# A second plain block that also makes the sums of weights; seven products in three blocks instead of four

## What is computed

```python
for t in range(S):
    state = gamma * state + einsum('bhd,bhe->bhde', k[:, :, t], v[:, :, t])
    y[:, :, t] = scale * einsum('bhd,bhde->bhe', q[:, :, t], state)
x = y as (3072, 512)
h = x @ w_in                      # 512 -> 2048
g = where(h >= 1, h, where(h <= -1, 0, (h + 1)**2 / 4))
x = g @ w_out                     # 2048 -> 512
h = x @ w_in2                     # 512 -> 1024
ln = layernorm(h * softmax(h)) * g_ln
out = ln @ w_out2                 # 1024 -> 512
```

## Time and profile before

| | |
|---|---|
| median of 3 runs | 903.12 us |
| the profiled execution | 901.88 us |
| span of its instructions | 900.1 us |
| mean granted TensorE clock | 0.979 of full |
| TensorE matmul busy | 855.7 us, 95% |
| VectorE busy | 578.3 us, 64% |
| ScalarE busy | 355.6 us, 40% |
| GpSimd busy | 270.9 us, 30% |

### The profile page before, as it was taken

The page is one execution under the profiler, slowest core; times in us unless marked ns, Lnnn a source line. Parts: engine busy times, 40 slices in busy tenths (PEclk is TensorE's granted clock), DMA queues, the critical chain, the costliest instruction groups (busy, mean ns, idle before and its releaser), DMA issues.

```text
span 900.1 us, 14076 instructions
## 1 busy us (share of the span) xinstructions
PE 855.7 (95%) x5392; PEld 729.3 (81%) x5392; DVE 578.3 (64%) x1046; ACT 355.6 (40%) x557; POOL 270.9 (30%) x244
## 2 busy tenths in 40 slices
PE   9978975999999998999989999999999999999998
PEld 7766764888888887888878887888877888888886
DVE  5677765554675457645575554367788889888841
ACT  3343332222242223322242223336466766767541
POOL 3534534222432234222431212224621311122000
PEclk9999996999999999999999999999999999999999
DMA  9944562443444343544333430421044465545452
GB/s 350 378 164 149 165 210 92 167 139 120 141 126 142 120 143 103 156 150 141 121 120 120 132 117 1 141 94 48 0 164 153 147 190 171 181 130 170 144 166 70
DMA packets 75587, 129.13 MB, mean 143 GB/s; under 512 B 7552, under 2 KB 25984, under 8 KB 75520
## 3 DMA queue, kind: packets, MB, share of 16 engines
q1 hardware_dynamic: 75232, 127.97, 43.9%
q10 hardware_dynamic: 288, 0.26, 0.1%
HBM read 94.65 MB, written 33.55 MB: 142 GB/s over the span
## 4 chain that ended last, share of the span: by engine, by line
PE 71%; DVE 15%; ACT 5%; issue 4%; SPq 2%; DMA 2%; POOL 1%; ACTq 0%; DVEq 0%; POOLq 0%
PE acc L622 22%; PE h L530 18%; PE o_ps L1399 13%; PE p L1299 10%; PE h L592 3%; DVE x_lo L874 2%; PE att L473 2%; DVE g_raw L963 2%; PE att L484 2%; ACT g_raw L740 1%; DMA w_pair<-in_moe_w_in 1%; DVE s_raw L889 1%; PE att L508 1%; DVE g_raw L958 1%; SPq L298 1%
## 5 line engine op out<-in xcount | busy, mean ns | idle before, releaser
L622 PE MATMUL acc<-g_hi,w 128*128 128x512 f32 x768 | 259.0, 398 | 0.0
L1091 POOL TENSOR_TENSOR g_lo<-g_raw,g_hi 128x512 fp32r<-128x512 f32 x96 | 129.1, 1344 | 364.4 <-ACT g_hi L665 364.4
L622 PEld LDWEIGHTS acc<-g_hi,w 128*128 128x128 f32 x768 | 145.1, 189 | 35.3 <-issue 3.6
L971 DVE TENSOR_TENSOR h<-h 128x256 f32<-128x256 f32 x192 | 81.1, 423 | 130.8 <-PE h L530 92.0
L740 ACT ACTIVATE g_raw<-g_raw,half_bias 128x512 f32<-128x512 f32 x96 | 69.2, 720 | 237.4 <-DVE g_raw L958 237.4
L622 PE MATMUL acc<-g_lo,w 128*128 128x512 f32 x384 | 150.5, 392 | 0.0
L530 PE MATMUL h<-x_hi,s 128*128 128x256 f32 x512 | 98.1, 290 | 0.9 <-DVE g_raw L963 0.9
L665 ACT ACTIVATE g_hi<-g_raw 128x512 fp32r<-128x512 f32 x96 | 60.7, 633 | 94.5 <-DVE g_raw L963 94.5
L530 PE MATMUL h<-x_hi,w 128*128 128x256 f32 x384 | 73.8, 288 | 20.2 <-DVE x_lo L874 12.5
L530 PEld LDWEIGHTS h<-x_hi,s 128*128 128x128 f32 x512 | 84.8, 198 | 3.6 <-DVE g_raw L963 1.2
L963 DVE TENSOR_TENSOR g_raw<-h,g_raw 128x512 f32<-128x512 f32 x96 | 68.8, 717 | 25.2 <-ACT g_raw L740 25.2
(11 more groups left out here) (140 smaller groups left out, 1512.2 us busy)
## 6 DMA issues: line engine op xcount, KB each, us to landing
s<-w_sums SPq DMA_DIRECT2D x128, 256.0 KB, 2.7
z<-zq SPq DMA_DIRECT2D x24, 512.0 KB, 2.8
zt<-z SPq DMA_DIRECT2D x94, 128.0 KB, 3.1
kT<-in_kT SPq DMA_DIRECT2D x24, 256.0 KB, 3.0
q<-in_q SPq DMA_DIRECT2D x24, 256.0 KB, 2.9
v<-in_v SPq DMA_DIRECT2D x24, 256.0 KB, 3.6
x2T<-y SPq DMA_DIRECT2D x24, 256.0 KB, 3.0
x_raw<-x2T SPq DMA_DIRECT2D x12, 512.0 KB, 4.9
```

The costliest lines, as they stand in the source:

```text
L622: last = mm(acc[m][:, :], ww, gg[:, f % 2, :], start=f == 0 and t == 0, stop=f == FT1 - 1 and t == 2)
L971: tt(out, of_product(p), other, ALU.add).then_inc(sem["taken1"], 1)
L1091: tt(g[1][:, f % 2, :], gate[:, f % 2, :], g[0][:, f % 2, :].bitcast(F32), ALU.subtract)\
```

## The change

Block 1 becomes a second plain block. The making of the sums of weights moves from block 0 to it, in steps 0, 1, 3, 4, 6, 7, 9 and 10 (the low parts in the steps after), and the SyncE queue is reordered to match; `store_x2(0)` stands in it ahead of the first `store_sums`. Blocks 2, 3 and 4 keep the seven products. In a pair, product 7 comes before product 6. `X_ORDER[0]`, the order of splits at the change to the first seven-product block, is t3, t2, t4, b11, b21, t1, b22. At the change from one seven-product block to the next, ScalarE copies b11 and b21 before it copies the high part of the previous activation; VectorE subtracts t3 after `larger` and no longer ahead of the joins of products 5 and 3; GpSimd makes t1 directly behind t3. At the change to block 5 (and to block 1) the four quarters of y are split by `split_y(blk, kt)` among the last step's work and no longer behind all of it.

```diff
-SEVEN = range(1, BLOCKS - 1)
+SUMS_BLOCK = 1
+SEVEN = range(SUMS_BLOCK + 1, BLOCKS - 1)
-P_ORDER = (1, 2, 6, 7, 5, 3, 4)
+P_ORDER = (1, 2, 7, 6, 5, 3, 4)
-PREPARE_AT = (2, 4, 5, 7, 8, 10, 11, 13)
+PREPARE_AT = (0, 1, 3, 4, 6, 7, 9, 10)
...
@@ SyncE @@
+            for c in range(B + 1, 2 * B + 1):
+                load_kT(c)
+                load_rest(c)
+            load_pair(0)
+            load_pair(1)
+            store_x2(0)
+            for b in range(B):
+                if b:
+                    load_kT(2 * B + b)
+                    load_pair(2 * b + 1)
+                    load_rest(2 * B + b)
+                store_sums(2 * b)
+                if b < B - 1:
+                    load_pair(2 * b + 2)
+                store_sums(2 * b + 1)
...
@@ TensorE, pair @@
+                have("t3")
+                product(7, sums(0), "t3")
                 have("t2")
-                product(6, sums(0), "t2")
-                have("t3")
-                product(7, sums(1), "t3")
+                product(6, sums(1), "t2")
...
@@ ScalarE, pair @@
+                if more:
+                    split_part(blk + 1, "b11")
+                    split_part(blk + 1, "b21")
                 if q:
                     high(*divmod(blk * FT1 + f - 1, FT1))
                 if more:
-                    for name in ("b11", "b21", "t3"):
-                        split_part(blk + 1, name)
+                    split_part(blk + 1, "t3")
+                if last:
+                    split_y(blk + 1, 0)
+                    split_y(blk + 1, 1)
                 square(blk, f)
+                if last:
+                    split_y(blk + 1, 2)
+                    split_y(blk + 1, 3)
...
@@ VectorE, pair @@
                 if more:
-                    for name in ("b11", "b21", "t3"):
-                        split_part(blk + 1, name)
+                    split_part(blk + 1, "b11")
+                    split_part(blk + 1, "b21")
                 join(q, 5, part, part, 3)
...
+                if last:
+                    split_y(blk + 1, 0)
                 larger(blk, f)
+                if last:
+                    for kt in range(1, KT):
+                        split_y(blk + 1, kt)
                 if more:
-                    split_part(blk + 1, "t2")
-                    split_part(blk + 1, "t1")
+                    for name in ("t3", "t2", "t1"):
+                        split_part(blk + 1, name)
...
@@ VectorE, dense: at the change to the first block with seven products @@
+                    if change:
+                        for name in X_ORDER[0][:4]:
+                            split_part(blk + 1, name)
                     clamp(blk, f)
+                    if change:
+                        split_part(blk + 1, X_ORDER[0][4])
                     larger(blk, f)
+                    if change:
+                        for name in X_ORDER[0][5:]:
+                            split_part(blk + 1, name)
-                    if blk == 0:
-                        if f in PREPARE_AT:
-                            sums_of_weights(PREPARE_AT.index(f))
+                    if blk == SUMS_BLOCK:
                         if f - 1 in PREPARE_AT:
                             sums_low(PREPARE_AT.index(f - 1))
+                        if f in PREPARE_AT:
+                            sums_of_weights(PREPARE_AT.index(f))
...
@@ GpSimd, pair @@
                 if more:
                     sum_of_x(blk + 1, "t3")
+                    sum_of_x(blk + 1, "t1")
                 if q:
                     low(*divmod(blk * FT1 + f - 1, FT1))
                 if more:
-                    sum_of_x(blk + 1, "t1")
                     sum_of_x(blk + 1, "t2")
```

More of the change, by code:

```diff
@@ L60, in made, with pair_number @@
     return len(P_ORDER) * q + P_ORDER.index(product) + 1
+def pair_number(blk, p):
+    return (blk - SEVEN[0]) * FPAIRS + p
 def h_count(blk, f):
-    return (FT1 if blk else 0) + f + 1
+    return min(blk, SEVEN[0]) * FT1 + f + 1
 def x_parts(blk):
-    return 0 if blk == 0 else 7 * blk if blk in SEVEN else 7 * len(SEVEN) + KT
+    return sum(7 if n in SEVEN else KT for n in range(1, blk + 1))
 X_ORDER = (("t3", "t2", "t4", "b11", "b21", "t1", "b22"), ("b11", "b21", "t3", "t2", "t1", "b22", "t4"))
 def x_made(blk, part):
-    return x_parts(blk - 1) + X_ORDER[min(blk - 1, 1)].index(part) + 1
+    return x_parts(blk - 1) + X_ORDER[min(blk - SEVEN[0], 1)].index(part) + 1
 def steps(blk):
@@ L580, in up @@
                 n = blk * FT1 + f
-                if blk and f < 2:
+                if blk > SEVEN[0] and f < 2:
                     pe.wait_ge(sem["taken1"], 7 * LAST_Q)
@@ L653, in _ @@
                 outputs(c)
-            dense(0)
+            for blk in range(SEVEN[0]):
+                dense(blk)
             for blk in SEVEN:
@@ L751, in dense @@
                 for f in range(steps(blk)):
-                    if blk == 0 and f == FT1 - 1:
-                        for name in X_ORDER[0]:
-                            split_part(1, name)
+                    if f == FT1 - 1 and blk + 1 < SEVEN[0]:
+                        for kt in range(KT):
+                            split_y(blk + 1, kt)
+                    if f == FT1 - 1 and blk + 1 == SEVEN[0]:
+                        for name in X_ORDER[0][:-1]:
+                            split_part(blk + 1, name)
                     if f == LAG - 1 and blk:
@@ L757, in dense @@
                     square(blk, f)
+                    if f == FT1 - 1 and blk + 1 == SEVEN[0]:
+                        split_part(blk + 1, X_ORDER[0][-1])
                     high(blk, f)
@@ L762, in dense @@
                         split_w_out(f)
[L763 to L764 removed]
+                    if blk == SUMS_BLOCK and f in PREPARE_AT:
+                        sums_high(PREPARE_AT.index(f))
                     if blk == BLOCKS - 1:
@@ L768, in pair @@
             def pair(blk, p):
-                q = (blk - 1) * FPAIRS + p
+                q = pair_number(blk, p)
                 f = 2 * p
                 more = blk + 1 in SEVEN and p == FPAIRS - 1
+                last = blk + 1 not in SEVEN and p == FPAIRS - 1
                 if p == 1:
@@ L872, in split_part, with split_y @@
                 if name == "t2":
-                    dve.wait_ge(sem["x_summed"], 4 * blk)
+                    dve.wait_ge(sem["x_summed"], 4 * (blk - SEVEN[0]) + 4)
                 tt(x_part(name, 1), x_raw(name), x_part(name, 0).bitcast(F32), ALU.subtract)\
                     .then_inc(sem["x_lo"], 1)
[L877 to L881, removed]
+            def split_y(blk, kt):
+                dve.wait_ge(sem["x_hi"], x_parts(blk - 1) + kt + 1)
+                tt(x[1][:, kt, :], y[:, kt, :], x[0][:, kt, :].bitcast(F32), ALU.subtract)\
+                    .then_inc(sem["x_lo"], 1)
             def sums_of_weights(i):
@@ L988, in pair @@
                 join(q, 7, part7, part, 2)
-                if p == 0 and blk > 1:
+                if p == 0 and blk > SEVEN[0]:
                     split_part(blk, "b22")
@@ L1018, in dense @@
                 for f in range(steps(blk)):
-                    if blk == 0 and f == FT1 - 1:
-                        for name in X_ORDER[0]:
-                            split_part(1, name)
+                    change = f == FT1 - 1 and blk + 1 == SEVEN[0]
+                    if f == FT1 - 1 and blk + 1 < SEVEN[0]:
+                        for kt in range(KT):
+                            split_y(blk + 1, kt)
+                    if change:
+                        for name in X_ORDER[0][:4]:
+                            split_part(blk + 1, name)
                     if blk < BLOCKS - 1:
```

104 lines of the change are left out of this document (40 added, 64 removed).

## The result

The changed kernel takes 865.49 us (median of 4 runs, 863.58 to 866.03) where the kernel before took 903.07 beside it: ratio 0.958, 95% interval 0.9563 to 0.9596. The forecast was 863, range 857 to 873. The profiled execution took 863.58 us, 38.3 less than that of before; its span is 861.7 us at a clock of 0.998.

A forecast was written before the change was run, and what follows sets the result against it. TensorE was taken as the bound nearly everywhere, with its standstills in the first 555 us to be won. Terms summed to -40.0 us from the profiled 901.88, giving 861.9; with 1.2 for the median, 863 us, range 857 to 873.

The forecast's parts named there:

- Block 0: Block 0 without the sums: TensorE becomes the bound, down 13 ends at 114.4 us instead of 131.70, -17.3 us.
- Change to block 1: From block 0 to block 1, now plain to plain: the old loss goes, 0.5 us of wait remains, -16.1 us.
- Block 1: Block 1 as a plain block: eight pairs at 5.44 us instead of 4.98, the sums costing nothing, +3.7 us.
- The room of 2 us per triple: VectorE in block 1: three steps need 17.9 us, under TensorE's 19.97, leaving 2 us of slack.
- Change to block 2: From plain to seven products: 2.8 us lost, no clock fall, the old 4.0 us stall gone, -1.2 us.
- Changes to blocks 3 and 4: Changes 2 to 3 and 3 to 4: 0.4 us each instead of 4.0, no first-product wait, -7.2 us together.
- the rule of exclusion: At changes 2 to 3 and 3 to 4, VectorE's max might wait for GpSimd's t1: about 0.4 us more each.
- Change to block 5: First quarters of y split before larger: the 2.17 us wait goes, 0.3 may remain at the third, -1.9 us.
- A: Rival: VectorE stays the bound in block 1, each of three triples costing 5.5 us, 879.5 us; chance 0.09.
- B: Rival: reordering at block changes doesn't do its part, another link ends as late, 872 us; chance 0.08.
- D: Rival: the single w_pair buffer is exposed, eight loads waited for in full, 905 us; chance 0.02.
- C: Rival: the last-split wait moves to the change to block 2, about 13 us instead of 2.8, 873 us; chance 0.05.

The follow-up runs named there:

- sums_in_0: The changed kernel with the sums of weights made in block 0 at the old steps, two plain blocks and new orders kept: 884.44 us, ratio 0.9789.
- more_work: The changed kernel with eight idle additions on VectorE ahead of each pair's sums in block 1: 879.71 us, ratio 0.9733.
- b_first: The changed kernel with b11 and b21 split first at the change to block 2, t3 between clamp and max: 862.40 us, ratio 0.9545.
- old_orders: The changed kernel with its block plan kept but every order inside a pair as in the kernel before: 872.10 us, ratio 0.9653.
- reorder_only: The changed kernel with the new orders kept but the block plan, sums and SyncE list of the kernel before: 890.91 us, ratio 0.9857.
- old_places_queue: The changed kernel with block 1's sums at the old step numbers and SyncE's list rewritten for those steps: 874.04 us, ratio 0.9678.
- old_places: The changed kernel with block 1's sums at the old step numbers, SyncE's list left alone: 908.19 us, ratio 1.0046.
- combo: The changed kernel with b11 and b21 first at block 2, two early y quarters at block 5, a later w_out copy at block 1: 863.12 us.

## Why the prediction was right, point by point

**Block 0** (-17.3): right, -17.1. TensorE is busy all through it. sums_in_0 shows that the sums, not the weight splits alone, had set VectorE's pace.

**Change to block 1** (-16.1): right, -15.7; 0.8 us stayed for the 0.5 taken. (0.3 us of this term, the slow start of the old `down`, lies in the table's third stretch. The two terms together are -12.5 for -12.4.)

**Block 1** (+3.7): the cover held, no wait in it, and sums_in_0 shows that the sums cost it nothing. The size is 3.2: a `down` between products takes 2.75 us and not 2.72, so the pairs of before were a little dearer than 4.98 against 5.44 says. The room of 2 us per triple was too small by half (4 us by the changed kernel's trace and more_work). I had carried over durations of VectorE measured in block 0, where its operations ran beside GpSimd's splits of w_out; that this made the difference is argued from the traces and not tested by itself.

**Change to block 2** (-1.2): the term that was mis-sized, 0.0. The mechanism was as told, three t parts ahead of b11. But I had only t2's split slowed by GpSimd, at 1.3 us. t3's was slowed too (1.55) and t2's took 1.76, so b11 was ready 5.4 us behind `up` 15 and not 4.7, and the wait was 2.65 us, not 1.9. The clock then fell, which I had taken as not to happen. What I took from two waits (2.17 us without a fall, 2.58 with one) was not enough to say so either way: all other kernels that wait 2.6 to 2.7 us here or at a later change had the fall behind it, but more_work had none behind 2.62 us in block 1 and 2.66 at this change. No wait of 1 to 2.2 us in the first phase was followed by a fall in any trace; b_first, whose longest wait here is 1.11 us, kept the clock.

**Changes to blocks 3 and 4** (-3.6 each): -3.6 each; the first product waits for nothing. The sum is as forecast, though the 0.4 us that I left for t3 is a wait of 0.77 for t4, and the old wait was a little dearer than the 4.0. What was late next was t4, not t3 or t2. old_orders and reorder_only give the orders 6.6 and 11.9 us, the latter for one change more. The 0.4 us that the rule of exclusion could have added at the max did not come: it took 0.88 us (312.39), shorter than before, having got in between t3 and t1. The rule's price came at t4.

**Change to block 5** (-1.9): -1.2. The first quarter was on time, the fourth was not; three splits in a row took 2.99 us beside GpSimd's low part.

**The sum** (-40.0): -37.9 by the table. The changes to blocks 2 and 5 gave 1.9 us less than forecast, the others are off by 0.5 us at most, in both directions.

**Rivals.** A, B and D did not happen. C did not either, and old_places_queue shows what it would have cost with later steps: 8.5 us. The way to a slower kernel was one that I had not listed: SyncE's list. I had walked through it for `store_x2(0)`, found nothing due, and not priced it. old_places shows its price at 34 us.

Open: which part of the differences of a microsecond between medians of like kernels is real. In the profiled executions TensorE's first `up` begins at 14.84 us (before), 15.15 (after), 15.48 (b_first) and 15.99 (combo), behind waits for the first loads of q that sum to 0.5 to 1.6 us; that alone moves the ends by up to 1.2 us.

## What to carry to other kernels

When work is moved to another step, its lines in the DMA queue's list move with it, or the queue holds up loads that have nothing to do with it. Room on an engine is its idle time in a window of the place where the work goes, less what it waits for the answer to its own work (here ScalarE's square), and not a cycle measured elsewhere beside other neighbours. At a change of blocks, split first what the first product reads; what lies ahead of it on VectorE is paid for, and paid twice if the clock falls.

## What the runs showed of the hardware

VectorE's split of 128x512 takes 0.68 us alone and 1.5 to 1.8 beside a GpSimd subtraction of 1.3 us, even if GpSimd began only 0.06 us before; it ended 0.55 us behind it in three kernels. The granted clock fell behind a wait of 2.65 us and stayed at 0.50 for 2.7 us of matmuls (0.77 instead of 0.40 us for two). Behind waits of nearly the same length in more_work it fell once (2.61 us) and stayed up twice (2.62 and 2.66).
